# Attention batch 0 joined to a first MLP: the softmax constant as a column, the weights' low halves moved from GpSimd to VectorE

## Chip, cores, metric

One core of a Trainium2 chip runs the whole program. The metric is the device time of one execution in microseconds (us).

## What is computed

Pooled attention, then two MLPs on its output, in float32:

```
B, H, S, D = 8, 8, 576, 64          # Sp = S / 8 = 72
k_p = k.reshape(B, H, Sp, 8, D).mean(axis=3);  v_p = v.reshape(B, H, Sp, 8, D).mean(axis=3)
scores = (q @ k_p^T) / sqrt(D);  scores -= max(scores)
attn = exp(scores);  attn = attn / (sum(attn) + 1e-09)
x = (attn @ v_p) as 4608 x 512      # tokens x heads and head columns
h = relu(x @ w_in);   x = (h * h) @ w_out         # d_ff 2048
h = x @ w_in2;  g = h if h >= 1, 0 if h <= -1, else (h + 1)^2 / 4;  out = g @ w_out2
```

## The kernel before

Each float32 value of the MLPs is kept as a high part (rounded, `w_hi`) and a low part (the rest, `w_lo`), and every product is three matmul passes: high by high, high by low, low by high. Tokens go in nine chunks of 512 for each MLP. A chunk has 16 blocks f of 128 hidden columns: `hidden(f)` is twelve matmuls of 512 columns (4 blocks kd of the model width, 3 passes) into `ps_h`, then relu and square on ScalarE and VectorE with the split into `g_hl`, then `output(f)`, twelve matmuls into `ps_y`. `hidden` runs two blocks ahead of `output`. Attention of batch b+1 is done in slots between the matmuls of chunk b.

Batch 0 has nothing to hide behind, so the functions named `first_...` run it alone, ahead of chunk 0, as eight units u: head pair u // 2, half u % 2 of the queries. For one unit TensorE turns q (`first_turn_q`, L815) and for even u also pools and turns k; ScalarE copies both; TensorE makes scores (L833); VectorE takes maxima and subtracts them (`first_shift`, L681); ScalarE takes exp (L524); VectorE sums, adds the constant and multiplies by 8 in a 6-column TENSOR_SCALAR (L696) and takes the reciprocal; GpSimd scales (`first_scale`, L437); TensorE turns the probabilities (`first_turn_p`, L843); ScalarE copies them to `p_t` (L529), reordering columns; TensorE multiplies with v (`first_pv`, L857); ScalarE and VectorE split the result into x high and low (L534, L709). `keep_warm` (L810) is a matmul whose result nobody reads.

Every engine has its own order of instructions, written out by hand, and they meet only at semaphores. Around the end of batch 0:

- GpSimd adds up v (L421), scales units 0 to 6, subtracts the low halves of weight blocks 0 and 1 (`first_w_lo`, L442), then goes to batch 1's k (`pool_sum`, L447). Unit 7 is scaled by VectorE (`last_scale`, L703).
- ScalarE casts whole weight blocks of 1024 columns (`split_w`, L501; 512 of w_in, 512 of w_out) within units 5 to 7.
- TensorE runs the first matmuls of hidden blocks 0 and 1 between the last units (`first_hidden_hi`, `first_hidden_lo`, L936 and L944), then chunk 0.
- SP issues all loads in one queue; the load of weight block 4 waits until the staging slot of block 0 has been read.

```
            first_pv(NU - 3)
            pe.wait_ge(q_copied, NU - 1)
            first_hidden_hi(0, range(2))
            first_turn_p(NU - 2)
            first_pv(NU - 2)
            pe.wait_ge(shifted, NU - 1)
            first_hidden_hi(1, range(2))
            first_turn_p(NU - 1)
```

## Time and profile before

| | us |
|---|---|
| median of 3 runs | 1770.72 |
| lowest, highest | 1768.55, 1771.09 |
| the profiled execution | 1771.15 |
| its span, first to last instruction | 1769.4 |
| TensorE busy | 1751.3 (99%) |
| VectorE, ScalarE, GpSimd busy | 761.8, 553.7, 229.7 |

The profile is of one execution. TensorE's busy time counts pipelined matmuls, so it shows whether the engine had something to do, not how fast it did it. The stretch that the change touches is the first 55 us of the span. Idle time counts only where it holds TensorE up.

### The profile page before, as it was taken

To read this page: it belongs to the slowest core of one execution; us is meant where nothing else is said; L and a number is where in the kernel's file an instruction comes from. 1 tells how busy PE (TensorE), PEld (TensorE's weight loads), DVE (VectorE), ACT (ScalarE), POOL (GpSimd) and SP (SyncE) were. 2 spreads that over 40 slices of the span, in tenths; PEclk is the share of its full clock that TensorE was granted. 3 is DMA by queue.
4 is the path that set the end of the run, shared out by engine and by line. 5 is a ranking of instruction groups with operands and counts; after the bars stand their busy time and mean duration, and the time that the engine had idled before them with its cause. 6 is when DMAs were issued, how large, how long until landed. Compare 5 with 4: busy or idle time off the path is not lost.

```text
span 1769.4 us, 22412 instructions
## 1 busy us (share of the span) xinstructions
PE 1751.3 (99%) x8371; PEld 1413.9 (80%) x8371; DVE 761.8 (43%) x1211; ACT 553.7 (31%) x970; POOL 229.7 (13%) x254
## 2 busy tenths in 40 slices
PE   8999999999999999999999999999999999999999
PEld 6777777777777777778888788888888888888887
DVE  6664434444444443433235434343434343434343
ACT  5453333333333333332234322222222222222222
POOL 6332313223131231310000000000000000000000
PEclk8999999999999999999999999999999999999999
DMA  6453324242331423213035202020201020201000
GB/s 153 126 153 122 85 71 120 65 124 81 104 99 59 130 74 118 84 61 107 1 116 170 95 1 72 1 71 0 71 0 71 0 71 0 71 0 71 0 24 24
DMA packets 117062, 126.86 MB, mean 72 GB/s; under 512 B 40192, under 2 KB 72448, under 8 KB 116992
## 3 DMA queue, kind: packets, MB, share of 16 engines
q1 hardware_dynamic: 116992, 125.86, 23.1%
q8 instruction: 53, 0.87, 0.2%
q14 instruction: 17, 0.14, 0.0%
HBM read 80.74 MB, written 45.09 MB: 71 GB/s over the span
## 4 chain that ended last, share of the span: by engine, by line
PE 96%; DVE 2%; ACT 1%; issue 0%; DMA 0%; POOL 0%; SPq 0%; ACTq 0%
PE ps_h L931 44%; PE ps_y L968 44%; PE ps_a L882 2%; PE ps_a L906 2%; PE ps_a L919 2%; PE ps_a L896 1%; DVE sq_f L726 1%; DMA first_kv<-in_v 0%; PE ps_h L941 0%; ACT act_f L569 0%; PE ps_y L863 0%; PE ps_y L852 0%; DVE probs L664 0%; DVE stat L662 0%; POOL first_kv L434 0%
## 5 line engine op out<-in xcount | busy, mean ns | idle before, releaser
L931 PE MATMUL ps_h<-xc,w_hi 128*128 128x512 f32 x2288 | 715.1, 394 | 0.0
L931 PEld LDWEIGHTS ps_h<-xc,w_hi 128*128 128x128 f32 x2288 | 423.0, 188 | 93.4 <-issue 9.2
L931 PE MATMUL ps_h<-xc,w_lo 128*128 128x512 f32 x1144 | 446.7, 390 | 0.0
L968 PE MATMUL ps_y<-w_hi,g_hl 128*128 128x512 f32 x1152 | 379.6, 391 | 3.1 <-DVE stage L750 2.2
L968 PE MATMUL ps_y<-g_hl,w_hi 128*128 128x512 f32 x1152 | 366.3, 399 | 1.5 <-DVE g_hl L730 1.5
L726 DVE TENSOR_TENSOR sq_f<-act_f 128x512 f32<-128x512 f32 x144 | 111.4, 774 | 414.0 <-ACT act_f L569 414.0
L968 PEld LDWEIGHTS ps_y<-w_hi,g_hl 128*128 128x128 f32 x1152 | 217.1, 188 | 49.0 <-DVE stage L750 2.6
L968 PEld LDWEIGHTS ps_y<-g_hl,w_hi 128*128 128x128 f32 x1152 | 209.7, 188 | 57.2 <-issue 15.3
L576 ACT ACTIVATE act_f<-act_f,half_bias 128x512 f32<-128x512 f32 x144 | 104.2, 724 | 480.2 <-DVE act_f L737 480.2
L931 PEld LDWEIGHTS ps_h<-xc,w_lo 128*128 128x128 f32 x1144 | 214.5, 188 | 46.4
L968 PE MATMUL ps_y<-g_hl,w_lo 128*128 128x512 f32 x576 | 225.7, 392 | 0.0
L968 PE MATMUL ps_y<-w_lo,g_hl 128*128 128x512 f32 x576 | 224.6, 390 | 0.0
L737 DVE TENSOR_SCALAR act_f<-ps_h 128x512 f32<-128x512 f32 x144 | 99.4, 690 | 252.3 <-PE ps_h L931 252.3
L569 ACT ACTIVATE act_f<-ps_h 128x512 f32<-128x512 f32 x144 | 86.0, 597 | 365.1 <-PE ps_h L931 363.3
L740 DVE TENSOR_TENSOR act_f<-ps_h,act_f 128x512 f32<-128x512 f32 x144 | 99.5, 691 | 113.8 <-ACT act_f L576 113.8
L743 DVE TENSOR_TENSOR g_hl<-act_f,g_hl 128x512 fp32r<-128x512 f32 x144 | 99.6, 692 | 98.7 <-ACT g_hl L579 98.7
L453 POOL TENSOR_TENSOR kv_raw<-kv_raw 72x512 f32<-72x512 f32 x112 | 119.5, 1067 | 115.0 <-DMA kv_raw<-in_k 110.7
L968 PEld LDWEIGHTS ps_y<-g_hl,w_lo 128*128 128x128 f32 x576 | 108.1, 188 | 24.6
L968 PEld LDWEIGHTS ps_y<-w_lo,g_hl 128*128 128x128 f32 x576 | 108.5, 188 | 22.5
L579 ACT CAST g_hl<-act_f 128x512 fp32r<-128x512 f32 x144 | 89.3, 620 | 109.0 <-DVE act_f L740 109.0
L730 DVE TENSOR_TENSOR g_hl<-sq_f,g_hl 128x512 fp32r<-128x512 f32 x144 | 108.4, 753 | 6.2 <-DVE sq_f L726 0.4
L470 POOL TENSOR_TENSOR probs<-probs,stat 96x432 f32<-96x432 f32 x56 | 52.8, 942 | 386.7 <-DVE stat L679 386.7
(81 smaller groups left out, 945.9 us busy)
## 6 DMA issues: line engine op xcount, KB each, us to landing
mlp_out_hl<-stage SPq DMA_DIRECT2D x36, 512.0 KB, 4.3
xc<-mlp_out_hl SPq DMA_DIRECT2D x36, 512.0 KB, 5.7
xc<-attn_out_hl SPq DMA_DIRECT2D x32, 512.0 KB, 3.9
attn_out_hl<-xo_hl SPq DMA_DIRECT2D x56, 288.0 KB, 2.3
out<-stage SPq DMA_DIRECT2D x36, 256.0 KB, 2.1
stage<-in_moe_w_in SPq DMA_DIRECT2D x32, 256.0 KB, 3.6
stage<-in_moe_w_out SPq DMA_DIRECT2D x32, 256.0 KB, 4.7
kv_raw<-in_k SPq DMA_DIRECT2D x28, 288.0 KB
```

Of the source, the lines that this page charges most:

```text
L453: nc.gpsimd.tensor_tensor(raw[:, :, 0:width], raw[:, :, 0:width], raw[:, :, width:2 * width], ALU.add).then_inc(kv_add, 1)
L470: nc.gpsimd.tensor_tensor(groups(probs[:, u % 2, :]), groups(probs[:, u % 2, :]), row_stat(u % 2, 3), ALU.mult).then_inc(probs_ready, 1)
L569: nc.scalar.activation(act_f[:, f % 2, :], ps_h[:, f % 2, :], ACT.Relu).then_inc(relu_done, 1)
L576: nc.scalar.activation(act_f[:, f % 2, :], act_f[:, f % 2, :], ACT.Square, bias=half_bias[:, 0:1], scale=0.5).then_inc(ramp_done, 1)
L579: nc.scalar.copy(g_hl[:, f % 2, 0, :], act_f[:, f % 2, :]).then_inc(g_hi_done, 1)
L726: nc.vector.tensor_tensor(sq_f[:, f % 2, :], act_f[:, f % 2, :], act_f[:, f % 2, :], ALU.mult).then_inc(square_done, 1)
L730: nc.vector.tensor_tensor(g_hl[:, f % 2, 1, :], sq_f[:, f % 2, :], g_hl[:, f % 2, 0, :].bitcast(F32), ALU.subtract).then_inc(g_ready, 1)
L737: nc.vector.tensor_scalar(act_f[:, f % 2, :], ps_h[:, f % 2, :], 1.0, -1.0, ALU.min, ALU.max).then_inc(clip_done, 1)
L740: nc.vector.tensor_tensor(act_f[:, f % 2, :], ps_h[:, f % 2, :], act_f[:, f % 2, :], ALU.max).then_inc(bend_done, 1)
L743: nc.vector.tensor_tensor(g_hl[:, f % 2, 1, :], act_f[:, f % 2, :], g_hl[:, f % 2, 0, :].bitcast(F32), ALU.subtract).then_inc(g_ready, 1)
L931: mm = nc.tensor.matmul(ps_h[:, f % 2, :], left[:, f, kd * P:(kd + 1) * P], xc[:, buf, right, kd, :], start=(kd == 0 and n == 0), stop=(kd ...
L968: mm = nc.tensor.matmul(ps_y[:, m, :], left, right, start=(f == 0 and n == 0), stop=(f == NF - 1 and n == 2))
```

## The change

- The constant stands as a 73rd column in each group of `first_p`, written once by GpSimd; the sum on VectorE runs over 73 columns, and the TENSOR_SCALAR of the eight units of batch 0 is gone. The factor 1/8 goes into ScalarE's copy to `p_t`.
- TensorE's transposes of probabilities write PSUM with a step of three columns, and ScalarE's copy reads and writes straight on.
- GpSimd scales unit 0 ahead of the second v, scales unit 7 too, does no w_lo, and goes on to batch 1's k.
- w_hi and w_lo of weight blocks 0 to 2 are made in halves of 512 columns by ScalarE and VectorE, the w_in halves ahead of the w_out halves, counted in `w_first_hi` and `w_first`.
- k of head pair 0 is loaded ahead of q and pooled ahead of turning q; there is one warm-up matmul more in three places.
- TensorE's matmuls of hidden block 0 come ahead of `first_pv(5)`, those of block 1 ahead of `first_pv(6)`; the last block's passes are reordered; the first half of hidden block 2 comes ahead of `output(0)`.

```diff
-              nc.sbuf_tensor("first_p", [QT, 3, GRP * SP_], F32) as first_p):
+              nc.sbuf_tensor("first_p", [QT, 3, GRP, SP_ + 1], F32) as first_p):
...
-                if 4 <= n < 6:
-                    sp.wait_ge(w_first, n - 3)
-                elif n >= 6:
-                    sp.wait_ge(w_ready, n - 5)
+                if 4 <= n < 7:
+                    sp.wait_ge(w_first, n)
+                elif n >= 7:
+                    sp.wait_ge(w_ready, n - 6)
...
+            first_load_k(0)
             first_load_q(0)
-            first_load_k(0)
...
+            nc.gpsimd.memset(first_p[:, :, :, SP_:SP_ + 1], EPS).then_inc(eps_set, 1)
...
             def first_scale(u):
                 pool.wait_ge(recip_done, u + 1)
-                nc.gpsimd.tensor_tensor(groups(first_p[:, u % 3]), groups(first_p[:, u % 3]), row_stat(u % 2, 3),
+                nc.gpsimd.tensor_tensor(first_p[:, u % 3, :, 0:SP_], first_p[:, u % 3, :, 0:SP_], row_stat(u % 2, 3),
                                         ALU.mult).then_inc(first_probs, 1)
-
-            def first_w_lo(n):
-                pool.wait_ge(w_hi_done, n + 1)
-                nc.gpsimd.tensor_tensor(w_lo[:, n, :], stage[:, n, :], w_hi[:, n, :].bitcast(F32),
-                                        ALU.subtract).then_inc(w_first, 1)
...
-            for hp in range(2):
-                for i in range(3):
-                    first_add_v(hp, i)
+            for i in range(3):
+                first_add_v(0, i)
             first_scale(0)
+            first_add_v(1, 0)
             first_scale(1)
+            first_add_v(1, 1)
+            first_add_v(1, 2)
+            first_scale(2)
             first_add_v(2, 0)
-            first_scale(2)
+            first_scale(3)
             first_add_v(2, 1)
-            first_scale(3)
             first_add_v(2, 2)
+            first_scale(4)
             first_add_v(3, 0)
-            first_scale(4)
+            first_scale(5)
             first_add_v(3, 1)
-            first_scale(5)
             first_add_v(3, 2)
             first_scale(6)
-            first_w_lo(0)
-            first_w_lo(1)
+            first_scale(7)
...
+            def first_split_w(n, half):
+                part = slice(half * DM, (half + 1) * DM)
+                act.wait_ge(w_loaded[n], 2 * DMA)
+                nc.scalar.copy(w_hi[:, n, part], stage[:, n, part]).then_inc(w_first_hi, 1)
...
             def first_copy_q(u):
+                if u == 0:
+                    act.wait_ge(k_turned, 1)
+                    copy_k(first_q_bank(1))
                 act.wait_ge(q_turned, u + 1)
                 copy_q(first_q_bank(u))
-                if u % 2 == 0:
+                if u and u % 2 == 0:
                     act.wait_ge(k_turned, u // 2 + 1)
-                    copy_k(first_q_bank(u + 1))
+                    copy_k(first_q_bank(1))
...
             def first_copy_p(u):
                 act.wait_ge(probs_turned, u + 1)
-                nc.scalar.copy(p_t[:].rearrange("n a (p j) -> n a j p", j=NJ),
-                               ps_y[0:SP_, 0:2, 0:HALF].rearrange("n a (j p) -> n a j p", j=NJ)).then_inc(p_copied, 1)
+                nc.scalar.activation(p_t[:], ps_y[0:SP_, 0:2, 0:HALF], ACT.Copy, scale=1.0 / POOL).then_inc(p_copied, 1)
...
+                    if layer == 1 and c.at(0) and f == 0:
+                        first_split_w(2, 1)
...
-                if u >= 5:
-                    split_w(u - 5)
+                if u >= NU - 2:
+                    first_split_w(u - NU + 2, 0)
             first_x_hi(NU - 3)
             first_copy_p(NU - 2)
             first_x_hi(NU - 2)
             first_copy_p(NU - 1)
+            first_split_w(2, 0)
             first_x_hi(NU - 1)
+            for n in range(2):
+                first_split_w(n, 1)
...
-                                        ALU.add).then_inc(sum_done, 1)
+                if u == 0:
+                    dve.wait_ge(eps_set, 1)
+                nc.vector.tensor_reduce(stat[:, u % 2, 1, :], first_p[:, u % 3], AX_X, ALU.add).then_inc(sum_done, 1)
                 dve.wait_ge(sum_done, u + 1)
-                nc.vector.tensor_scalar(stat[:, u % 2, 2, :], stat[:, u % 2, 1, :], EPS, float(POOL),
-                                        ALU.add, ALU.mult).then_inc(eps_done, 1)
-                dve.wait_ge(eps_done, u + 1)
                 if u >= 2:
                     dve.wait_ge(first_probs, u - 1)
-                nc.vector.reciprocal(stat[:, u % 2, 3, :], stat[:, u % 2, 2, :]).then_inc(recip_done, 1)
-
-            def last_scale():
-                u = NU - 1
-                dve.wait_ge(recip_done, u + 1)
-                nc.vector.tensor_tensor(groups(first_p[:, u % 3]), groups(first_p[:, u % 3]), row_stat(u % 2, 3),
-                                        ALU.mult).then_inc(last_probs, 1)
+                nc.vector.reciprocal(stat[:, u % 2, 3, :], stat[:, u % 2, 1, :]).then_inc(recip_done, 1)
+
+            def first_w_lo(n, half):
+                part = slice(half * DM, (half + 1) * DM)
+                dve.wait_ge(w_first_hi, 3 * half + n + 1)
+                nc.vector.tensor_tensor(w_lo[:, n, part], stage[:, n, part], w_hi[:, n, part].bitcast(F32),
+                                        ALU.subtract).then_inc(w_first, 1)
...
+                    if layer == 1 and c.at(0) and f == 0:
+                        first_w_lo(2, 1)
...
-                if u >= 3:
+                if 3 <= u < NU - 1:
                     first_x_lo(u - 3)
             first_sums(NU - 1)
-            last_scale()
+            first_x_lo(NU - 4)
             first_x_lo(NU - 3)
+            first_w_lo(0, 0)
+            first_w_lo(1, 0)
             first_x_lo(NU - 2)
-            split_w(2)
+            first_w_lo(2, 0)
             first_x_lo(NU - 1)
+            first_w_lo(0, 1)
+            first_w_lo(1, 1)
...
-                if u == NU - 1:
-                    pe.wait_ge(last_probs, 1)
-                else:
-                    pe.wait_ge(first_probs, u + 1)
+                pe.wait_ge(first_probs, u + 1)
...
                 for a in range(2):
                     for j in range(NJ):
-                        mm = nc.tensor.transpose(ps_y[0:SP_, a, j * QT:(j + 1) * QT],
-                                                 first_p[:, u % 3, (2 * j + a) * SP_:(2 * j + a + 1) * SP_],
+                        mm = nc.tensor.transpose(ps_y[0:SP_, a, 0:HALF].rearrange("n (p j) -> n j p", j=NJ)[:, j, :],
+                                                 first_p[:, u % 3, 2 * j + a, 0:SP_],
                                                  ident[0:QT, 0:QT])
                 mm.then_inc(probs_turned, 1)
...
+            def first_hidden(f, left, right, blocks, start=False, stop=False):
+                for kd in blocks:
+                    mm = nc.tensor.matmul(ps_h[:, f, :], left[:, f, kd * P:(kd + 1) * P], xc[:, 0, right, kd, :],
+                                          start=(start and kd == blocks[0]), stop=stop)
+                if stop:
+                    mm.then_inc(h_ready, 1)
 
...
+                if c.at(0) and f < 3:
+                    pe.wait_ge(w_first, f + 4)
...
+                        hidden(c, buf, f + 2, weights, [2, 3] if fixed == 0 and f == 0 else range(KD))
...
+            first_pool_k(0)
             first_turn_q(0)
-            keep_warm(2)
+            keep_warm(3)
             first_scores(0)
             first_turn_q(1)
-            keep_warm(1)
+            keep_warm(2)
             for u in range(NU - 1):
                 first_scores(u + 1)
                 if u + 2 < NU:
                     first_turn_q(u + 2)
+                if u % 2 == 0 and u + 2 < NU:
+                    first_pool_k(u // 2 + 1)
                 if u < 2:
-                    keep_warm(2)
+                    keep_warm(2 + u)
                 if u >= 2:
                     first_pv(u - 2)
                 if u >= 1:
                     first_turn_p(u - 1)
+            pe.wait_ge(q_copied, NU - 1)
+            first_hidden_hi(0, [0, 1])
             first_pv(NU - 3)
-            pe.wait_ge(q_copied, NU - 1)
-            first_hidden_hi(0, range(2))
             first_turn_p(NU - 2)
+            pe.wait_ge(shifted, NU - 1)
+            first_hidden_hi(1, [0, 1])
             first_pv(NU - 2)
-            pe.wait_ge(shifted, NU - 1)
-            first_hidden_hi(1, range(2))
             first_turn_p(NU - 1)
             for f in range(2):
                 first_hidden_hi(f, [2])
             first_pv(NU - 1)
             for f in range(2):
-                first_hidden_lo(f, range(KD - 1))
-            for f in range(2):
-                first_hidden_hi(f, [KD - 1])
-                first_hidden_lo(f, [KD - 1])
+                first_hidden_lo(f, [0, 1, 2])
+            pe.wait_ge(x_hi_done, NU)
+            first_hidden(0, w_hi, 0, [KD - 1])
+            first_hidden(0, w_lo, 0, [KD - 1])
+            pe.wait_ge(x_split, NU)
+            first_hidden(0, w_hi, 1, [KD - 1], stop=True)
+            first_hidden(1, w_hi, 0, [KD - 1])
+            first_hidden(1, w_lo, 0, [KD - 1])
+            first_hidden(1, w_hi, 1, [KD - 1], stop=True)
+            pe.wait_ge(relu_done, 1)
+            hidden(At(0), 0, 2, 0, [0, 1])
```

GpSimd's start of batch 0, before (`first_kv` is raw v, `v_sum` its sum, `first_p` the probabilities of a unit):

```order
L434 TENSOR_TENSOR first_kv<-first_kv 72x2x256 [waits v_first0]
L434 TENSOR_TENSOR first_kv<-first_kv 72x2x128 [waits first_add]
L431 TENSOR_TENSOR v_sum<-first_kv 72x128 [waits first_add]
L434 TENSOR_TENSOR first_kv<-first_kv 72x2x256 [waits v_first1]
L434 TENSOR_TENSOR first_kv<-first_kv 72x2x128 [waits first_add]
L431 TENSOR_TENSOR v_sum<-first_kv 72x128 [waits first_add]
L439 TENSOR_TENSOR first_p<-first_p,stat 96x432 [waits recip_done] x2
L434 TENSOR_TENSOR first_kv<-first_kv 72x2x256 [waits v_first2]
L439 TENSOR_TENSOR first_p<-first_p,stat 96x432 [waits recip_done]
```

and of the change:

```order
L436 TENSOR_TENSOR first_kv<-first_kv 72x2x256 [waits v_first0]
L436 TENSOR_TENSOR first_kv<-first_kv 72x2x128 [waits first_add]
L433 TENSOR_TENSOR v_sum<-first_kv 72x128 [waits first_add]
L441 TENSOR_TENSOR first_p<-first_p,stat 96x6x72 [waits recip_done]
L436 TENSOR_TENSOR first_kv<-first_kv 72x2x256 [waits v_first1]
L441 TENSOR_TENSOR first_p<-first_p,stat 96x6x72 [waits recip_done]
L436 TENSOR_TENSOR first_kv<-first_kv 72x2x128 [waits first_add]
L433 TENSOR_TENSOR v_sum<-first_kv 72x128 [waits first_add]
L441 TENSOR_TENSOR first_p<-first_p,stat 96x6x72 [waits recip_done]
L436 TENSOR_TENSOR first_kv<-first_kv 72x2x256 [waits v_first2]
```

The first scaling moved ahead of the second v, and each further v's additions behind the scaling of an earlier unit.

VectorE from the sum of unit 7 to the first square, before (`xc` is x low, `xo_hl` its tail):

```order
L693 TENSOR_REDUCE stat<-first_p 96x6 [waits exp_done]
L696 TENSOR_SCALAR stat<-stat 96x6 [waits sum_done]
L701 RECIPROCAL stat<-stat 96x6 [waits first_probs,eps_done]
L706 TENSOR_TENSOR first_p<-first_p,stat 96x432 [waits recip_done]
L717 TENSOR_TENSOR xc<-ps_y,xc 128x224 [waits x_hi_done]
L719 TENSOR_TENSOR xo_hl<-ps_y,xo_hl 128x64
L713 TENSOR_TENSOR xc<-ps_y,xc 128x288 [waits x_hi_done]
L653 TENSOR_TENSOR w_lo<-stage,w_hi 128x1024 [waits w_hi_done]
L717 TENSOR_TENSOR xc<-ps_y,xc 128x224 [waits x_hi_done]
L719 TENSOR_TENSOR xo_hl<-ps_y,xo_hl 128x64
L726 TENSOR_TENSOR sq_f<-act_f 128x512 [waits relu_done]
```

and of the change:

```order
L705 TENSOR_REDUCE stat<-first_p 96x6 [waits exp_done]
L709 RECIPROCAL stat<-stat 96x6 [waits first_probs,sum_done]
L721 TENSOR_TENSOR xc<-ps_y,xc 128x288 [waits x_hi_done]
L725 TENSOR_TENSOR xc<-ps_y,xc 128x224 [waits x_hi_done]
L727 TENSOR_TENSOR xo_hl<-ps_y,xo_hl 128x64
L714 TENSOR_TENSOR w_lo<-stage,w_hi 128x512 [waits w_first_hi] x2
L721 TENSOR_TENSOR xc<-ps_y,xc 128x288 [waits x_hi_done]
L714 TENSOR_TENSOR w_lo<-stage,w_hi 128x512 [waits w_first_hi]
L725 TENSOR_TENSOR xc<-ps_y,xc 128x224 [waits x_hi_done]
L727 TENSOR_TENSOR xo_hl<-ps_y,xo_hl 128x64
L714 TENSOR_TENSOR w_lo<-stage,w_hi 128x512 [waits w_first_hi] x2
L734 TENSOR_TENSOR sq_f<-act_f 128x512 [waits relu_done]
```

The TENSOR_SCALAR and the last scaling are gone, and five half subtractions of w_lo stand where one whole one stood.

TensorE at units 5 to 7, before (L863 and L875 are v products, L852 and L864 transposes of probabilities):

```order
L863 MATMUL ps_y<-p_t,v_sum 64x288 [waits x_split,first_v_pooled,p_copied]
L863 MATMUL ps_y<-p_t,v_sum 64x288
L941 MATMUL ps_h<-xc,w_hi 128x512 [waits x_split,w_hi_done,q_copied]
L941 MATMUL ps_h<-xc,w_hi 128x512
L852 MATMUL ps_y<-ident,first_p 72x96 [waits p_copied,first_probs]
L852 MATMUL ps_y<-ident,first_p 72x96 x5
L863 MATMUL ps_y<-p_t,v_sum 64x288 [waits x_split,first_v_pooled,p_copied]
L863 MATMUL ps_y<-p_t,v_sum 64x288
L941 MATMUL ps_h<-xc,w_hi 128x512 [waits x_split,w_hi_done,shifted]
```

and of the change:

```order
L864 MATMUL ps_y<-ident,first_p 72x96 [waits p_copied,first_probs]
L864 MATMUL ps_y<-ident,first_p 72x96 x5
L952 MATMUL ps_h<-xc,w_hi 128x512 [waits x_split,w_first_hi,q_copied]
L952 MATMUL ps_h<-xc,w_hi 128x512 x3
L875 MATMUL ps_y<-p_t,v_sum 64x288 [waits x_split,first_v_pooled,p_copied]
L875 MATMUL ps_y<-p_t,v_sum 64x288
L864 MATMUL ps_y<-ident,first_p 72x96 [waits p_copied,first_probs]
L864 MATMUL ps_y<-ident,first_p 72x96 x5
L952 MATMUL ps_h<-xc,w_hi 128x512 [waits x_split,w_first_hi,shifted]
```

The four w_hi matmuls of hidden block 0 moved ahead of the product of unit 5, block 1's ahead of that of unit 6.

## Rows read from the trace of the kernel before

**Rows 1.** The page: TensorE's busy time and share, and the chain by engine.
```profile
PE 1751.3 (99%) x8371; PEld 1413.9 (80%) x8371; DVE 761.8 (43%) x1211; ACT 553.7 (31%) x970; POOL 229.7 (13%) x254
...
PE 96%; DVE 2%; ACT 1%; issue 0%; DMA 0%; POOL 0%; SPq 0%; ACTq 0%
```

**Rows 2.** TensorE's timeline: start us, us, engine, line, operation, idle before and releaser.
```profile
14.77 0.73 PE L812 MATMUL ps_y<-warm 128*128 128x512 f32 x2
16.63 0.69 PE L852 MATMUL ps_y<-ident,first_p 96*72 96x96 f32 x6 [1.12 <-POOL first_p L439]
...
22.61 0.69 PE L852 MATMUL ps_y<-ident,first_p 96*72 96x96 f32 x6
...
28.59 0.69 PE L852 MATMUL ps_y<-ident,first_p 96*72 96x96 f32 x6
29.11 0.90 PE L839 MATMUL ps_a<-k_bd,q_t 128*96 128x144 f32 x6
30.79 0.71 PE L863 MATMUL ps_y<-p_t,v_sum 72*64 72x288 f32 x4 [0.78 <-ACT p_t L531]
...
33.25 1.23 PE L863 MATMUL ps_y<-p_t,v_sum 72*64 72x288 f32 x4 [1.13 <-ACT p_t L531]
...
38.46 1.23 PE L863 MATMUL ps_y<-p_t,v_sum 72*64 72x288 f32 x4 [1.01 <-ACT p_t L531]
...
49.12 0.73 PE L968 MATMUL ps_y<-g_hl,w_hi 128*128 128x512 f32 x2 [1.46 <-DVE g_hl L730]
...
66.75 0.66 PE L919 MATMUL ps_a<-ident,probs 96*72 96x96 f32 x6 [1.44 <-DVE probs L664]
```

**Rows 3.** Windows: busy of PE, PEld, DVE, ACT, POOL; granted clock; DMA; GB/s.
```profile
29.00:33.00 4.00, 2.34 (x20) 1.45 (x17) 3.49 (x11) 4.00 (x8) 1.69 (x3) 1.00 0.45 93
33.00:43.50 10.50, 9.24 (x31) 5.92 (x32) 8.07 (x8) 4.12 (x8) 10.27 (x8) 0.51 0.04 9
```

**Rows 4.** GpSimd's timeline, 13 to 66 us.
```profile
13.10 2.07 POOL L434 TENSOR_TENSOR first_kv<-first_kv 72x512 f32<-72x512 f32 x2
...
15.67 0.91 POOL L439 TENSOR_TENSOR first_p<-first_p,stat 96x432 f32<-96x432 f32 x1
...
33.50 4.68 POOL L444 TENSOR_TENSOR w_lo<-stage,w_hi 128x1024 fp32r<-128x1024 f32 x2
...
40.54 1.57 POOL L460 TENSOR_TENSOR k_sum<-kv_raw 72x128 f32<-72x128 f32 x1
...
52.36 0.46 POOL L460 TENSOR_TENSOR k_sum<-kv_raw 72x128 f32<-72x128 f32 x1 [8.21 <-PE ps_a L892]
62.30 0.91 POOL L470 TENSOR_TENSOR probs<-probs,stat 96x432 f32<-96x432 f32 x1 [9.48 <-DVE stat L679]
63.17 2.86 POOL L453 TENSOR_TENSOR kv_raw<-kv_raw 72x512 f32<-72x512 f32 x2
```

**Rows 5.** VectorE's timeline, 34 to 66 us.
```profile
34.26 3.95 DVE L696 TENSOR_SCALAR stat<-stat 96x6 f32<-96x6 f32 x1
...
47.64 0.69 DVE L726 TENSOR_TENSOR sq_f<-act_f 128x512 f32<-128x512 f32 x1 [1.88 <-ACT act_f L569]
...
62.47 1.28 DVE L726 TENSOR_TENSOR sq_f<-act_f 128x512 f32<-128x512 f32 x1 [0.25 <-ACT act_f L569]
63.79 1.66 DVE L730 TENSOR_TENSOR g_hl<-sq_f,g_hl 128x512 fp32r<-128x512 f32 x1
```

**Rows 6.** ScalarE's groups by shape: count | busy us, mean ns | idle before.
```profile
L579 ACT CAST g_hl<-act_f 128x512 fp32r<-128x512 f32 x144 | 89.3, 620 | 109.0 <-DVE act_f L740 109.0
...
L564 ACT COPY p_t<-ps_a 72x576 f32<-72x576 f32 x56 | 35.2, 629 | 22.7 <-PE ps_a L919 22.7
...
L531 ACT COPY p_t<-ps_y 72x576 f32<-72x576 f32 x8 | 7.6, 948 | 7.7 <-PE ps_y L852 7.5
```

**Rows 7.** TensorE's weight loads, timeline at 6 us.
```profile
6.07 1.07 PEld L828 LDWEIGHTS ps_a<-ident,first_kv 72*64 72x64 f32 x32 [0.42 <-DMA first_kv<-in_k]
```

**Rows 8.** The chain that ended last, in order of time: start us, us, what.
```profile
55.98 2.77 PE ps_y L968 x12
```

61 lines of the change are left out of this document (28 added, 33 removed).

## The prediction

> **What bounds the kernel now.** I read the busy shares first: TensorE is busy 1751.3 of 1769.4 us and makes up 96% of the chain that ended last [rows 1]. So nothing that another engine does counts unless TensorE waits for it. Then TensorE's timeline over the first 70 us, looking for gaps [rows 2]. Batch 0's attention has three parts. Up to 16.63 us it fills; the first transposes of probabilities start then, 1.12 us late, waiting for GpSimd. From 16.63 to 29.8 us TensorE has no gap: two units (u = 2, 3) take 28.59 - 22.61 = 5.98 us whatever the others do. From 29.85 us on it drains, with gaps of 0.78, 1.13, 1.01 and 1.46 us until the first product of the output matmul starts at 49.12. The only gap behind that in chunk 0 that I find is 1.44 us at 66.75. The windows [rows 3] show the second loss of the drain: between 29 and 33 us TensorE is busy 2.34 of 4 us at full clock, and from 33.0 to 43.5 us the granted clock is 0.51, the lower level (1.2 GHz). It fell after the gaps of 0.78 and 1.13 us, and rose once the matmuls stood close again.
>
> The cause on the other engines: VectorE's 6-column TENSOR_SCALAR at 34.26 takes 3.95 us [rows 5], exactly until GpSimd ends its two w_lo subtractions, 33.50 to 38.18 [rows 4]. The last unit's probabilities stand behind it. ScalarE meanwhile copies p_t in 0.95 us a time [rows 6], between w_hi casts of 1024 columns.
>
> **The start.** GpSimd ends batch 0's first v at 13.10 to 13.14 us, but starts the scaling of unit 0 only at 15.67, behind the second v [rows 4]. Now it scales at once: done at 13.14 + 0.91 = 14.05. Then TensorE itself decides: its two warm-ups at 14.77 end issue at 14.77 + 2 x 0.23 = 15.23, and the change adds one, 15.46. The loads give something back: k's first matmul waited at 6.07 for its load, with q already turned [rows 7]; now k is loaded and pooled first, and q, the last to land, is followed by 0.65 us of turning and 0.40 of copying instead of 1.17 and 0.45. That is worth 0 to 0.6 us; I take 0.3, since q's pieces may land a little after k's did. The other added warm-up stands in a wait for ScalarE's copy, so it costs nothing; if that copy were early it would cost 0.23. First transposes at 15.16 instead of 16.63: **1.47 us**. The close stretch carries this shift unchanged. On GpSimd the second v now ends near 17.8, and its first reader (unit 2's product) starts near 23.
>
> **The drain**, laid out by hand from the rows, all at full clock. Transposes of unit 4 at 27.12 (28.59 before). Steps on TensorE: 0.52 us for six transposes (28.59 to 29.11), 0.84 for scores and 0.55 for a pv pair (busy 0.90 and 0.71, less the overlap with what follows [rows 2]), 0.23 for a matmul of 512 columns (twelve take 2.77 [rows 8]). On ScalarE p_t's copy is now contiguous: 0.65 instead of 0.95, after the 0.63 of batch 1's same copy [rows 6]; a w_hi half is 0.60, after the 0.62 of a cast of 512 columns [rows 6]. On VectorE the constant as a 73rd column removes the TENSOR_SCALAR (0.17 to 3.95 us) from all eight units. pv(4) starts at 28.54 and transposes(5) at 29.10; the four w_hi matmuls of block 0 now stand between them and pv(5) and fill the gap: 29.62 to 30.56. pv(5) 30.56. Transposes(6) need exp(6) 29.03, sum 30.34, reciprocal 30.53, scaling by GpSimd 31.49: start 31.54, a gap of 0.43. Block 1's four matmuls 32.06 (before 39.62), pv(6) 32.99, transposes(7) 33.54, scaling(7) by GpSimd having ended at 32.85. Then four w_hi matmuls 34.06, pv(7) 34.99, six w_lo 35.54, and the last six to 38.3. Relu(0) 37.84 to 38.44. The first half of hidden block 2 (six matmuls, 1.39 us), formerly behind the first output, fills 38.49 to 39.88.
>
> **What the moved work costs.** Five half w_lo subtractions and GpSimd's batch-1 additions now fall between 32.8 and 42 us. Where a TENSOR_TENSOR of VectorE meets a GpSimd instruction, the rows show one waiting for the other: the square at 62.47 takes 1.28 instead of 0.69 while GpSimd scales until 63.2; the subtraction at 63.79 takes 1.66 while GpSimd adds; and GpSimd's k_sum takes 1.57 instead of 0.46 under VectorE's w_lo [rows 4, 5]. They take turns. With additions of 1.26 and 0.80 (2.07 a pair), 0.46, and 1.26 and 0.80 again [rows 4], in turn with halves of 0.66 us (a little under the 0.69 of a square of 512 columns [rows 5]): w_lo(0) is ready at 33.5, w_lo(1) 35.4 (needed 36.2), w_lo(2) 36.9 (needed 38.5), output half 0 at 38.0, output half 1 at 39.9. Then square(0) waits out GpSimd's last addition, 40.73, and ends at 41.42, g_lo(0) at 42.11: first output matmul at 42.16. Without any turns, g_lo(0) would come at 38.49 + 0.69 + 0.72 = 39.9 and the output at 40.0. So the turns cost 2.2 us there, in the largest wait left.
> The Trainium skill (SBUF — State Buffer, section Who interferes with whom) says that a VectorE instruction with two SBUF inputs contends with a GpSimd instruction that reads SBUF, the first holding the port for its whole length, and that a reduce never does. It speaks against moving w_lo to VectorE without a hold on GpSimd; the traced 1.28, 1.66 and 1.57 us agree, and the reduces and reciprocals keep their length.
>
> **Sum.** The first output starts at 42.16 instead of 49.12, 6.96 us earlier (1.47 from the start, 5.49 from the drain), with 1.39 us of hidden block 2 already done: **8.35 us**. From there the same work follows in the same order. The wait at 66.75 comes from scores, maxima and the square held by GpSimd, all counted from TensorE's own start of output(1), so it should stay. Loads of weights 4 to 6 now wait for w_first, ready from 38.0 on, and SP reaches them only behind the x stores, which wait for unit 7's x split, now 37.3: nothing. The kernel's own profiled execution took 1771.15 us (span 1769.4): 1762.8. The median shown is 0.43 lower, 1770.72, so the forecast is **1762.4 us**.
>
> **Unknown prices.** ScalarE's copy with a factor: 0.63 to 0.95 us [rows 6]; at 0.95 the first output is at 42.76, 0.6 us later. Transposes that write PSUM with a step of three: no row has it. From below nothing, or a little less; from above, the nearest row is ScalarE's stepped copy, 0.95/0.63 = 1.5 times, which on 0.52 us for eight units is 2.1 us. I take nothing, since the step changes no count of columns, and keep 2.1 for the range. Turns between the two engines: from 0 (first output near 40.0, 2.2 us more gain) to the hold below.
>
> **The rivals.**
> 1. *The clock still falls in the drain* (0.14). For: it fell before after gaps of 0.78 and 1.13 us, and one of some 2.1 us stays in front of the first output. Against: every other gap is at most 0.43, and the 1.46 us gap before 49.12 came at full clock. If it ran at the lower level over the whole 30 to 40 us, some 5 us of matmuls would take twice as long: gain 3.4, 1767.4. If only behind the last gap, 2 to 3 us are lost: 1765.
> 2. *The hold comes back in another form* (0.12): GpSimd's additions follow one another as its two w_lo did, and VectorE is held over all five (4.6 us, to 38.1). For: the 3.95 us. Against: the additions wait for each other and let VectorE in (63.17 to 66.03). w_lo(1) at 38.7, first output near 42.9: 1763.2.
> 3. *The start gives nothing* (0.08): q lands later, or a load after it, and TensorE reaches unit 0's transposes only at 16.6: 1763.9.
> 4. *The stepped PSUM write is dear* (0.12), the case on the other side. It stands in the close stretch, where each of 48 transposes counts. At k times the price the loss is 4.2 (k - 1) us: 1764.5 at 1.5 times; at 3 times (a step of three costing what the span of columns does) the whole gain is gone, 1770.8; beyond 3.9 times it is slower than now by over 0.2%. For: ScalarE pays for a step. Against: TensorE passes columns one by one.
>
> **How the numbers follow.** The forecast has 0.54; its own range is 1760.0 (no turns) to 1764.5. 0.2% is 3.5 us, about what a measurement tells here. Faster by more: forecast 0.54, hold 0.12, start 0.08, clock 0.10 of 0.14, stepped write 0.04 of 0.12: 0.88. Within: 0.04 + 0.03 = 0.07. Slower: 0.05. The range, 1759.5 to 1767.0, reaches over the hold, the start and most of the clock, and leaves out the dear write and a drain wholly at the lower clock.
>
> **What would show it.** Right: first transposes of p near 15.2; no TENSOR_SCALAR on VectorE before batch 1; granted clock 1.0 throughout 33 to 43; p_t copies of 0.65; w_lo halves up to 1.9 us long beside GpSimd; six L944 matmuls before the first output, and that output near 42.2 behind a wait of about 2 us for g_hl. Wrong: six transposes over 0.6 us (rival 4), a clock row under 1 (rival 1), a w_lo half over 3 us (rival 2), first transposes at 16.6 (rival 3), or a gap behind the first output larger than the 1.44 us at 66.75.

## The result, and the profile after

| us | before | after |
|---|---|---|
| median (lowest, highest; executions) | 1770.89 (1768.55, 1772.47; 8) | 1763.77 (1762.58, 1765.52; 8) |
| profiled execution, its span | 1771.15, 1769.4 | 1764.07, 1762.3 |
| TensorE busy | 1751.3 | 1747.7 |

The change makes the kernel 0.4% faster: ratio 0.9962, 95% interval [0.9953, 0.9971], 7.1 us by the medians. The forecast was 1762.4 us, 1.4 us too low; the range of 1759.5 to 1767.0 holds the result.

The page of the kernel after, TensorE's busy time and the chain by engine, to be put beside [rows 1]:

```profile
PE 1747.7 (99%) x8374; PEld 1411.7 (80%) x8374; DVE 760.3 (43%) x1207; ACT 552.0 (31%) x973; POOL 226.6 (13%) x254
...
PE 97%; DVE 2%; issue 0%; ACT 0%; POOL 0%; ACTq 0%; POOLq 0%
```

TensorE's timeline of the kernel after (start us, us, engine, line, operation, count, idle before and releaser), to be put beside [rows 2]:

```profile
15.42 0.66 PE L864 MATMUL ps_y<-ident,first_p 96*72 96x96 f32 x6
...
27.35 0.69 PE L864 MATMUL ps_y<-ident,first_p 96*72 96x96 f32 x6
...
29.89 1.17 PE L952 MATMUL ps_h<-xc,w_hi 128*128 128x512 f32 x4
30.99 0.71 PE L875 MATMUL ps_y<-p_t,v_sum 72*64 72x288 f32 x4
31.84 0.69 PE L864 MATMUL ps_y<-ident,first_p 96*72 96x96 f32 x6
...
34.04 0.69 PE L864 MATMUL ps_y<-ident,first_p 96*72 96x96 f32 x6
...
39.29 0.73 PE L944 MATMUL ps_h<-xc,w_hi 128*128 128x512 f32 x2
...
41.39 0.70 PE L985 MATMUL ps_y<-g_hl,w_hi 128*128 128x512 f32 x2 [0.44 <-DVE g_hl L738]
...
57.62 0.66 PE L931 MATMUL ps_a<-ident,probs 96*72 96x96 f32 x6 [1.44 <-DVE probs L674]
...
383.75 0.66 PE L931 MATMUL ps_a<-ident,probs 96*72 96x96 f32 x6 [1.35 <-DVE probs L674]
```

Windows of the kernel after (busy of PE, PEld, DVE, ACT, POOL; granted clock; DMA; GB/s), to be put beside [rows 3]:

```profile
29.00:33.00 4.00, 3.86 (x27) 2.40 (x24) 3.42 (x10) 3.48 (x9) 3.16 (x5) 1.00 0.21 51
33.00:43.50 10.50, 10.05 (x48) 6.58 (x47) 9.95 (x14) 7.08 (x14) 6.13 (x6) 1.00 0.22 65
```

The drain is closed: the w_hi matmuls of block 0 (29.89) stand where TensorE waited 1.13 us, the granted clock is 1.00 where it was 0.51, and TensorE waits 0.44 us in front of the first output. The row at 57.62 is the same work as the one at 66.75 in [rows 2], with the same wait of 1.44 us. By there 66.75 - 57.62 = **9.13 us** are gained: 1.21 in front of the first transposes of p (16.63 against 15.42), and 7.92 between the two marks (50.12 us before, 42.20 after). I call this stretch, from the first transposes of p to batch 1's first transposes of probs, the **drain mark**. The end has only 1771.15 - 1764.07 = 7.08 us of the 9.13: **2.05 us are given back later**, in two steps. Against the same rows of before, the kernel after is 9.09 us ahead at its row at 274.69, 8.29 at the one at 383.75, where the wait is 1.35 us instead of 0.59, 7.03 at the one at 601.58, and between 7.02 and 7.08 from there to the end.

GpSimd's timeline of the kernel after, beside [rows 4]:

```profile
12.96 0.90 POOL L441 TENSOR_TENSOR first_p<-first_p,stat 96x432 f32<-96x432 f32 x1
...
33.05 2.86 POOL L450 TENSOR_TENSOR kv_raw<-kv_raw 72x512 f32<-72x512 f32 x2
35.99 0.97 POOL L457 TENSOR_TENSOR k_sum<-kv_raw 72x128 f32<-72x128 f32 x1
36.93 2.44 POOL L450 TENSOR_TENSOR kv_raw<-kv_raw 72x512 f32<-72x512 f32 x2
```

VectorE's timeline of the kernel after, beside [rows 5]:

```profile
32.79 2.53 DVE L714 TENSOR_TENSOR w_lo<-stage,w_hi 128x512 fp32r<-128x512 f32 x2
...
37.38 2.53 DVE L714 TENSOR_TENSOR w_lo<-stage,w_hi 128x512 fp32r<-128x512 f32 x2
39.84 0.68 DVE L734 TENSOR_TENSOR sq_f<-act_f 128x512 f32<-128x512 f32 x1
...
374.52 0.69 DVE L734 TENSOR_TENSOR sq_f<-act_f 128x512 f32<-128x512 f32 x1 [5.60 <-issue]
```

The scaling of unit 0 starts right behind the first v (12.96). Pairs of w_lo halves take 2.53 us beside the additions. The last row is new: 5.60 us in which VectorE waited for nothing that the profile shows; the square at the same place before, at 382.06, stands behind ScalarE's relu (4.40 us idle). The page's rows for the queues of instruction fetches (queue: packets, MB, share), first of before, then of after:

```profile
q14 instruction: 17, 0.14, 0.0%
```

```profile
q14 instruction: 27, 0.22, 0.0%
```

The ten more packets all lie between 367 and 800 us, five from 367 on and five from 583 on, at the loop's two ways back; before has none there.

### The profile page after: what moved, and what is told of

Read it like the earlier page. It is cut to its first block, busy times and chain, and to the rows that moved or that the text cites. A ratio compares the mean times of both kernels' runs of the same rounds, so it can differ in the third digit from the quotient of the medians.

```text
span 1762.3 us, 22444 instructions
## 1 busy us (share of the span) xinstructions
PE 1747.7 (99%) x8374; PEld 1411.7 (80%) x8374; DVE 760.3 (43%) x1207; ACT 552.0 (31%) x973; POOL 226.6 (13%) x254
## 4 chain that ended last, share of the span: by engine, by line
PE 97%; DVE 2%; issue 0%; ACT 0%; POOL 0%; ACTq 0%; POOLq 0%
PE ps_h L944 44%; PE ps_y L985 44%; PE ps_a L894 2%; PE ps_a L918 2%; PE ps_a L931 2%; PE ps_a L908 1%; DVE sq_f L734 1%; PE ps_y L826 0%; PE ps_a L843 0%; DVE probs L674 0%; PE ps_y L864 0%; ACT act_f L574 0%; DVE stat L672 0%; PE ps_y L875 0%; PE ps_h L854 0%
```

## The experiments

How they compare: how long TensorE's first matmuls run at half rate differs from execution to execution (last section) and moves everything behind them by up to 2.7 us, so single profiles are compared by the drain mark, and times by the ratio to the kernel before on the same chip. The three chips are those of a_body226, a_pad4, b_body234 and b_column; of a_pvfirst, a_hold, b_hifirst and b_colhi; and of b_wvec, b_wvechi, a_vfirst and a_nohid2. Medians of two chips are not compared closely.

One thing more moves the times, whatever the kernel. In front of the second MLP, near 980 us, TensorE waits 2.17 us in every profile. Behind this wait the granted clock falls for about 3.4 us in 12 of the 14 profiled executions, and not in those of a_body226 and a_nohid2; from there to the end TensorE takes 778.0 us with the fall (after: 977.95 to 1755.96) and 776.5 without (a_body226: 977.68 to 1754.14). Windows of after and of a_body226:

```profile
977.50:982.50 5.00, 4.55 (x13) 3.60 (x14) 3.53 (x7) 2.48 (x5) 0.00 (x0) 0.66 0.75 277
```

```profile
977.50:982.50 5.00, 4.82 (x21) 3.98 (x22) 3.52 (x7) 2.22 (x4) 0.00 (x0) 1.00 0.81 297
```

Of an execution without a profile only the mean granted clock over the whole kernel is known. In the profiled ones it is 0.996 with before's fall in the drain and this one (10 and 3 us), 0.998 with a fall of about 3.5 us in each place (b_hifirst), 0.999 with one fall of some 3 us, and 1.000 with none (a_body226).

| kernel | median us | ratio, 95% interval | first p | drain mark |
|---|---|---|---|---|
| before | 1770.7, 1771.3, 1771.6 (three chips) | | 16.63 | 50.12 |
| after | 1763.77 | 0.9962 [0.9953, 0.9971] | 15.42 | 42.20 |
| a_body226 | 1761.24 | 0.9950 [0.9937, 0.9962] | 17.34 | 42.24 |
| a_pad4 | 1763.21 | 0.9963 [0.9948, 0.9977] | 14.80 | 42.19 |
| a_pvfirst | 1763.58 | 0.9957 [0.9944, 0.9970] | 14.74 | 43.21 |
| a_hold | 1762.85 | 0.9952 [0.9938, 0.9966] | 17.42 | 42.71 |
| a_vfirst | 1763.16 | 0.9953 [0.9940, 0.9967] | 16.89 | 42.26 |
| a_nohid2 | 1763.63 | 0.9955 [0.9941, 0.9969] | 17.43 | 45.16 |
| b_body234 | 1771.97 | 1.0004 [0.9995, 1.0013] | 17.07 | 50.07 |
| b_column | 1771.04 | 0.9996 [0.9985, 1.0007] | 15.86 | 49.94 |
| b_hifirst | 1771.19 | 1.0001 [0.9992, 1.0011] | 16.53 | 49.19 |
| b_colhi | 1769.59 | 0.9989 [0.9977, 1.0000] | 18.44 | 49.33 |
| b_wvec | 1767.47 | 0.9979 [0.9970, 0.9988] | 16.67 | 46.58 |
| b_wvechi | 1765.73 | 0.9968 [0.9955, 0.9980] | 16.85 | 44.95 |

### Where 2 us went: the length of VectorE's loop

The diff touches one line of VectorE inside the loop: `b.times(NU, u + 1)` became `b.times(NU, u + 1 - NU)`, since batch 0 no longer counts eps_done. That value was shared with other waits; now it needs register instructions of its own. Counted in the program, the loop over chunks has 226 instructions on VectorE before and 234 after.

**a_body226**: the changed kernel, with the constant's memset counting for batch 0.

```diff
-            nc.gpsimd.memset(first_p[:, :, :, SP_:SP_ + 1], EPS).then_inc(eps_set, 1)
+            nc.gpsimd.memset(first_p[:, :, :, SP_:SP_ + 1], EPS).then_inc(eps_done, NU)
-                    dve.wait_ge(eps_set, 1)
+                    dve.wait_ge(eps_done, NU)
-                    dve.wait_ge(eps_done, b.times(NU, u + 1 - NU))
+                    dve.wait_ge(eps_done, b.times(NU, u + 1))
```

> The changed kernel, but the memset of the constant's column counts eps_done up to 8, so that the wait of batches 1 to 7 is again on the same register value as the others and the loop of VectorE has 226 instructions as before the change, instead of 234 (its start stays at instruction 152). Theory 1 (the longer loop body no longer fits what VectorE keeps, so its start is fetched again at each way back): the two late starts of VectorE at the second and third pass (5.60 us before the square at 374.5) are gone, the waits of TensorE there are 0.59 instead of 1.35, and the kernel is 1.6 to 2.2 us faster than the change: 1761.7. Theory 2 (the position of the loop's start, which the change moved from instruction 156 to 152): no difference, 1763.8. Theory 3 (the stores beside it slow the same fetch): no difference.

TensorE's timeline of a_body226 at the place of the row at 383.75, and its page's row for the fetches:

```profile
384.86 0.66 PE L930 MATMUL ps_a<-ident,probs 96*72 96x96 f32 x6 [0.59 <-DVE probs L673]
```

```profile
q14 instruction: 17, 0.14, 0.0%
```

The wait is back at 0.59 us, the fetches at 17, and the time is 1761.24 us: 9.5 us under before's median on that chip. Not all of the 2.5 us to after's median is the loop's: four of the six executions have a mean clock of 1.000 (1759.75 to 1762.22 us), the other two, with 0.999 like all eight of after, took 1762.49 and 1764.65. What the loop costs is read from the traces. **a_pad4** keeps 234 instructions and moves where the loop starts, by four memsets of one column ahead of it on VectorE:

```diff
+            for i in range(4):
+                nc.vector.memset(pad[:, i:i + 1], 0.0)
```

> The changed kernel with four memsets of one column each ahead of everything on VectorE, where it idles for 8 us: the loop starts at instruction 156 again, as before the change, and keeps its 234 instructions. Theory 1 (length of the body): the two late starts stay, 1763.8. Theory 2 (position of the start): they are gone, 1761.7.

It stays near after's time, with 27 fetch packets, as theory 1 had it; only the places moved (TensorE waits 0.33 and 1.32 us for the late q_t at 378.68 and 596.44). The waits of a_pad4, VectorE's (engine, line waited for: us in total, times, longest):

```profile
DVE g_hl L739 <- issue: 6.2, 2, 3.5
```

**b_body234** is the reverse: the kernel before, batch 0 counting on a semaphore of its own.

```diff
-                                        ALU.add, ALU.mult).then_inc(eps_done, 1)
-                dve.wait_ge(eps_done, u + 1)
+                                        ALU.add, ALU.mult).then_inc(eps_first, 1)
+                dve.wait_ge(eps_first, u + 1)
...
-                    dve.wait_ge(eps_done, b.times(NU, u + 1))
+                    dve.wait_ge(eps_done, b.times(NU, u + 1 - NU))
```

> The kernel before, with batch 0's TENSOR_SCALAR counted in a semaphore of its own, so that the loop of VectorE has 234 instructions instead of 226 and starts at 156 as before; nothing else. Theory 1: the two late starts appear here too and cost 1.6 to 2.2 us: 1772.7. Theory 2: no difference, 1770.8.

VectorE's waits in b_body234:

```profile
DVE stat L663 <- issue: 5.6, 2, 3.0
```

The late starts come, at the two ways back of the loop, with 27 packets, and TensorE waits 0.94 and 0.34 us for q_t there; the median is 1.2 us above before's, which its interval can't tell from nothing. The traces can: from batch 1's first transposes of probs to those of batch 7 (66.75 to 716.94 in before) TensorE takes 652.30, 651.66 and 651.43 us in the three kernels with 234 instructions, and 649.90 to 650.58 in ten of the eleven with 226; the eleventh, a_pvfirst, has 651.19, with 0.82 us of TensorE's own `issue` idle. So the eight instructions are the cause of the late starts in both kernels, and they cost 1 to 2 us, by what TensorE needs from VectorE just then. The Trainium skill (Runtime: NRT & Kernel Launch, section Instruction fetch mechanics) says that an engine's instruction memory holds two blocks, filled in sequence, and that a taken branch to a target outside of them waits for a fetch. The ten added packets and the 5.60 us at the loop's way back agree; that the step from 226 to 234 crosses such an edge is my reading, and no run measured where the edge lies.

### What closed the drain: the change in parts, on the kernel before

**b_column**: the constant as a column, with the factor in ScalarE's copy, and nothing else.

```diff
-                nc.vector.tensor_scalar(stat[:, u % 2, 2, :], stat[:, u % 2, 1, :], EPS, float(POOL),
-                                        ALU.add, ALU.mult).then_inc(eps_done, 1)
-                dve.wait_ge(eps_done, u + 1)
```

> The kernel before with the constant as a column alone: no TENSOR_SCALAR in batch 0, the factor 1/8 in ScalarE's copy (which still reorders columns), all orders as before, GpSimd's w_lo too. Theory A (the prediction's: VectorE's instruction held for 3.95 us is what makes the drain long): unit 7's probabilities come up to 3 us earlier and the first output starts 2 to 4 us earlier, 1767 to 1769. Theory B (it stood in the shadow of TensorE at the lower clock and of ScalarE's copies; unit 7's transposes at 41.49 waited for the matmuls ahead of them, not for the probabilities ready at 39.9): the first output moves by less than 0.5 us, 1770.5.

VectorE's timeline of b_column:

```profile
33.48 0.19 DVE L701 RECIPROCAL stat<-stat 96x6 f32<-96x6 f32 x1
33.70 3.97 DVE L706 TENSOR_TENSOR first_p<-first_p,stat 96x432 f32<-96x432 f32 x1
```

The held instruction is gone, and the next one is held in its stead, 3.97 us for 3.95, over GpSimd's w_lo subtractions (32.54 to 37.21). The reciprocal, which starts beside them too, takes its usual 0.19. The column alone is worth nothing beyond the start: theory B. The median hides two of the ten executions, 1765.68 and 1765.92 us, whose mean clock of 1.000 leaves room for neither of the two falls.

**b_hifirst**: the order of TensorE alone. **b_colhi**: both.

```diff
-            first_pv(NU - 3)
             pe.wait_ge(q_copied, NU - 1)
             first_hidden_hi(0, range(2))
+            first_pv(NU - 3)
...
-            first_pv(NU - 2)
             pe.wait_ge(shifted, NU - 1)
             first_hidden_hi(1, range(2))
+            first_pv(NU - 2)
```

> The kernel before with one thing of the change: the four w_hi matmuls of block 0 ahead of pv(5), those of block 1 ahead of pv(6). Theory 'order': the gaps of 1.13 and 1.01 us fill, units 5 and 6 come about 1 us each earlier; the transposes of unit 7 then wait in the open for VectorE's TENSOR_SCALAR held to 38.2 and its scaling to 39.9 (now 41.5): 1.6 to 2 us gained at full clock, and the wait of some 3.9 us shows as a gap. If the clock stays full up to there, what it costs (about 5 us, from the two runs of b_column that kept it) comes on top in part: 1764 to 1766; if the clock falls in the long gap instead, 1768 to 1769. Theory 'VectorE decides': no more than 1.6 us.

> The kernel before with the constant as a column (b_column) and the w_hi matmuls ahead of pv(5) and pv(6). In b_column the hold had passed from the TENSOR_SCALAR to the next instruction, the last scaling (TENSOR_TENSOR, 3.97 us, to 37.67), so that the column gained nothing but the start. Against b_hifirst the column now saves the TENSOR_SCALAR and the reciprocal behind the hold, 0.8 us of start and about 1.4 us of the scaling: unit 7's transposes at 37.7 instead of 39.9, 2 us more gained than b_hifirst (1762 to 1766). If w_lo on VectorE is what counts, the gap of 1.8 us in front of unit 7 stays, and the time stays 1.5 us or more above that of a_body226 (1761.2).

TensorE's timeline of b_hifirst:

```profile
35.67 0.71 PE L863 MATMUL ps_y<-p_t,v_sum 72*64 72x288 f32 x4 [0.23 <-ACT p_t L531]
39.84 1.07 PE L852 MATMUL ps_y<-ident,first_p 96*72 96x96 f32 x6 [3.46 <-DVE first_p L706]
40.62 2.05 PE L941 MATMUL ps_h<-xc,w_hi 128*128 128x512 f32 x4
```

The gaps of 1.13 and 1.01 us shrink to 0.17 and 0.23, and what they hid appears: one gap of 3.46 us for unit 7's probabilities, behind the held TENSOR_SCALAR. The clock falls behind it (four w_hi matmuls in 2.05 us; 1.17 in front of it), and nothing is left of the gain: 0.93 us at the drain mark, none in the median. In b_colhi the gap is 2.02 us, the clock falls all the same, and 1.7 us are gained by the median, at the edge of its interval. For b_hifirst the theory "VectorE decides" held; the 1762 to 1766 expected of b_colhi missed, and its other theory, that w_lo on VectorE is what counts, is the one that fits.

**b_wvec**: w_lo(0) and w_lo(1) on VectorE, nothing else. **b_wvechi**: that and the order of b_hifirst.

```diff
-                pool.wait_ge(w_hi_done, n + 1)
-                nc.gpsimd.tensor_tensor(w_lo[:, n, :], stage[:, n, :], w_hi[:, n, :].bitcast(F32),
+                dve.wait_ge(w_hi_done, n + 1)
+                nc.vector.tensor_tensor(w_lo[:, n, :], stage[:, n, :], w_hi[:, n, :].bitcast(F32),
...
             first_x_lo(NU - 3)
+            first_w_lo(0)
             first_x_lo(NU - 2)
+            first_w_lo(1)
             split_w(2)
```

> The kernel before with one thing of the change: w_lo(0) and w_lo(1) made by VectorE (whole, 1024 columns) and not by GpSimd, behind the last scaling and the split of unit 5's x; TensorE's order and the constant as before. Theory 'both together': the hold on the TENSOR_SCALAR (3.95 us) goes, but the gaps of 0.78 and 1.13 us in front of pv(4) and pv(5) stay, so the clock falls at about 33 us as before, and unit 7 comes only as far ahead as the doubled durations let it: gain 0 to 1 us, 1770.3 to 1771.3. Theory 'the hold was it': unit 7 comes as soon as its probabilities are there, the clock rises earlier: 2 to 4 us gained, 1767 to 1769.

> The kernel before with two things of the change: w_lo(0) and w_lo(1) on VectorE as in b_wvec, and the w_hi matmuls ahead of pv(5) and pv(6) as in b_hifirst. Theory 'both together': no gap over 0.8 us up to the last matmul of hidden block 1, granted clock 1.0 throughout, unit 7's transposes at about 36.3 instead of 39.8 in b_hifirst; the first output some 5 to 6 us ahead of before's: 1765 to 1766.5, below the sum of the two alone. Theory 'the column is needed too' (its TENSOR_SCALAR and reciprocal and the last scaling on VectorE stay in front of unit 7): under 3 us, 1768 or more.

TensorE's timeline of b_wvec:

```profile
30.85 0.71 PE L863 MATMUL ps_y<-p_t,v_sum 72*64 72x288 f32 x4 [0.79 <-ACT p_t L524]
...
33.30 0.71 PE L863 MATMUL ps_y<-p_t,v_sum 72*64 72x288 f32 x4 [1.13 <-ACT p_t L524]
33.94 1.20 PE L941 MATMUL ps_h<-xc,w_hi 128*128 128x512 f32 x4
...
36.65 0.71 PE L863 MATMUL ps_y<-p_t,v_sum 72*64 72x288 f32 x4 [1.02 <-ACT p_t L524]
```

Its windows, and VectorE's TENSOR_SCALAR of unit 7:

```profile
33.00:43.50 10.50, 8.86 (x46) 5.61 (x47) 8.43 (x12) 4.68 (x10) 7.65 (x6) 1.00 0.06 13
```

```profile
34.31 0.54 DVE L689 TENSOR_SCALAR stat<-stat 96x6 f32<-96x6 f32 x1
```

This part alone gives 4.1 of the 7.1 us: theory "the hold was it" (1767 to 1769), and not the 0 to 1 us of the other; but the clock didn't rise earlier in this profile, it never fell in the drain. The TENSOR_SCALAR takes 0.54 us, unit 7's scaling ends at 36.09 instead of 39.87, and TensorE goes through the **same three gaps** as before (0.79, 1.13, 1.02 us) with the clock at 1.00. A mean clock of 0.999 or more over the whole kernel, which leaves no room for before's fall of 10 us, stands in 9 of its 11 executions, and in 9 of the 64 of the kernel before (1 of 16 on the same chip). The two others of b_wvec took 1770.91 and 1771.61 us, hardly less than before's 1771.66 with the fall on that chip: the gain comes where the clock is kept. With the order on top the drain mark falls by another 1.63 us, and the median stands 5.9 us below before's, as "both together" had it; the order alone was worth nothing. So the parts don't add up one by one: the order pays once the hold on VectorE is gone, and the hold goes only with w_lo off GpSimd.

What else lies between b_wvechi (44.95) and after (42.20) is 2.75 us: 1.39 of it the half of hidden block 2, the rest the column, the contiguous copy, and w_lo in halves, which were not tried apart on this base.

### The parts taken out of the changed kernel

These four stand on a_body226. **a_pvfirst** puts pv(5) and pv(6) back in front of the w_hi matmuls:

```diff
-            first_hidden_hi(0, [0, 1])
             first_pv(NU - 3)
+            first_hidden_hi(0, [0, 1])
...
+            first_pv(NU - 2)
             pe.wait_ge(shifted, NU - 1)
             first_hidden_hi(1, [0, 1])
-            first_pv(NU - 2)
```

> The changed kernel with a_body226's form of the semaphore (so that the loop keeps its 226 instructions), and on TensorE the old order alone: pv(5) and pv(6) each ahead of the four w_hi matmuls that the change put in front of them. Theory 'order': these eight matmuls fill the waits for p_t's copy (TensorE has no gap over 0.2 us between 29 and 38 us in the changed kernel), and that keeps the granted clock at full. With the old order two gaps of 0.6 to 1.1 us come back (start times alone: about 1.2 to 1.5 us, 1762.6) and, if gaps decide the clock as in the kernel before, it falls to about 0.5 behind them, and costs some 5 us more: 1766 to 1768. Theory 'VectorE': what let the clock fall was the late last unit, behind GpSimd's w_lo; the order is worth its 1.2 to 1.5 us only, the clock stays 1.0: 1762.4 to 1762.8.

TensorE's timeline and a window of a_pvfirst:

```profile
30.21 0.71 PE L874 MATMUL ps_y<-p_t,v_sum 72*64 72x288 f32 x4 [0.78 <-issue]
...
33.27 0.71 PE L874 MATMUL ps_y<-p_t,v_sum 72*64 72x288 f32 x4 [0.74 <-ACT p_t L536]
```

```profile
33.00:43.50 10.50, 10.22 (x48) 7.02 (x49) 7.82 (x13) 7.09 (x14) 4.91 (x5) 1.00 0.22 65
```

Two gaps come back, cost 0.97 us at the drain mark, and the clock stays at 1.00 in this profile; none of the seven executions has a mean under 0.999, so none had a fall of 10 us. The order is worth its own gaps, and is not what holds the clock here: theory "VectorE" of the two, though its 1762.4 to 1762.8 was 1 us low.

**a_hold** gives GpSimd the hold that the change leaves out:

```diff
             first_scale(7)
+            pool.wait_ge(w_first, 5)
```

> The changed kernel with a_body226's form of the semaphore, and GpSimd waits for all five halves of w_lo of VectorE (w_first 5) before it goes on to batch 1's k. Theory of the prediction: the turns with GpSimd's additions cost 2.2 us in front of the first output; without them VectorE's pairs of w_lo take 1.4 instead of 2.53 us, the wait of TensorE in front of the first output goes, and the time falls by up to 2 us: 1759.2. Theory from the trace of after: only 0.44 us of TensorE's wait is left there, so at most 0.4 us is gained (1760.8); the additions, now from about 40.6 us on, meet the squares and g_lo instead, and may give that back and up to 1 us more (1762.2). Batch 1's k_sum at about 43 us stays ahead of TensorE's transpose of it (46 us).

VectorE's timeline of a_hold, and TensorE's first output:

```profile
39.39 1.29 DVE L714 TENSOR_TENSOR w_lo<-stage,w_hi 128x512 fp32r<-128x512 f32 x2
41.28 1.32 DVE L734 TENSOR_TENSOR sq_f<-act_f 128x512 f32<-128x512 f32 x1 [0.59 <-ACT act_f L574]
42.64 1.11 DVE L738 TENSOR_TENSOR g_hl<-sq_f,g_hl 128x512 fp32r<-128x512 f32 x1
```

```profile
43.89 0.70 PE L985 MATMUL ps_y<-g_hl,w_hi 128*128 128x512 f32 x2 [0.93 <-DVE g_hl L738]
```

The pair of halves takes 1.29 us alone instead of 2.53, but ends before relu(0) does, so that nothing is gained from it; the square and g_lo then meet the additions, 1.32 and 1.11 us instead of 0.68 and 0.69. The wait in front of the first output grows from 0.44 to 0.93, the drain mark by 0.47. In these two traces going on without a hold is right, by half a microsecond, and the turns in front of the first output cost at most 0.44 us. The median, 1762.85, lies above both forecasts; the ratios of the two kernels differ by 0.0002, far inside their intervals.

**a_vfirst** puts both first v ahead of the scaling of unit 0 on GpSimd again, as before:

```diff
-            first_scale(0)
-            first_add_v(1, 0)
-            first_scale(1)
-            first_add_v(1, 1)
-            first_add_v(1, 2)
+            for i in range(3):
+                first_add_v(1, i)
+            first_scale(0)
+            first_scale(1)
```

> The changed kernel with a_body226's form of the semaphore, and GpSimd's start as before: both first v ahead of the scaling of unit 0. Theory of the prediction: the scaling's place is what gives the start's gain, the first transposes of p wait 1.1 to 1.5 us again, and all behind them is that much later: 1762.3 to 1762.7 (a_body226: 1761.24). Rival: TensorE's own first 10 us, at half rate in some executions up to 10 us, make it reach the first transposes only at 17.3 us in those, so there GpSimd's order costs nothing, and over many executions less than half of it shows: 1761.3 to 1761.8.

TensorE's first transposes of p in a_vfirst:

```profile
16.89 0.69 PE L862 MATMUL ps_y<-ident,first_p 96*72 96x96 f32 x6 [1.30 <-POOL first_p L440]
```

In this execution TensorE's first microseconds are those of the profile of after (k's pooling 1.89 us in both), and the first transposes come 1.47 us later. The drain mark is unchanged (42.26). By the ratios it costs 0.0003, about 0.5 us, which is inside both intervals and decides between neither theory; the median lies above both (1763.16), but its 1.9 us to a_body226's are of two chips.

**a_nohid2** leaves hidden block 2 whole behind the first output:

```diff
-            pe.wait_ge(relu_done, 1)
-            hidden(At(0), 0, 2, 0, [0, 1])
...
-                        hidden(c, buf, f + 2, weights, [2, 3] if fixed == 0 and f == 0 else range(KD))
+                        hidden(c, buf, f + 2, weights)
```

> The changed kernel with a_body226's form of the semaphore, and hidden block 2 whole behind the first output, as before. Theory of the prediction: its first six matmuls (1.39 us) stand in a wait for g_hl and are a full gain; without them TensorE waits 0.44 + 1.39 = 1.83 us in front of the first output, which starts as now, and the rest is 1.39 us later: 1762.6. Rival: what follows waits for VectorE further on (the 1.44 us at 57.6 us of the changed kernel), and takes up the 1.39: 1761.2.

TensorE's timeline of a_nohid2:

```profile
43.40 0.70 PE L984 MATMUL ps_y<-g_hl,w_hi 128*128 128x512 f32 x2 [2.10 <-DVE g_hl L737]
...
45.07 1.05 PE L984 MATMUL ps_y<-g_hl,w_hi 128*128 128x512 f32 x2
```

The first output starts where it does in a_body226 (43.33), and the drain mark is 2.92 us longer: the 1.39 us of the six matmuls, and some 1.5 us because the granted clock fell behind the wait of 2.10 us (0.50 from 45 to 48). The median is 1 us above the 1762.6 of the first theory; against the rival speaks the trace, in which nothing up to batch 1 takes up the 1.39 us. So the half block fills a wait; that it also keeps the engine at its clock rests on this one profile. One of the five executions has a mean clock of 1.000 (1761.75 us), so the clock doesn't fall there each time.

## Why the prediction was right, and where it was off

- **Direction and size: right.** 8.35 us forecast, 7.08 measured between the two profiled executions.
- **The start**, 1.47 us forecast, 1.21 measured. GpSimd's scaling was out of the way as forecast; a_vfirst undoes this part and its first transposes come 1.47 us later at the same pace of TensorE's start. At the slower pace of a_body226 TensorE itself reaches them only at 17.34, so the gain isn't there in every execution. The 0.3 us hoped from loading k first went another way: q's turning was to take 0.65 us and k's pooling to lie ahead of it, but the pooling ran partly at half rate, 1.89 us for 1.22. In a_pad4, where it took 1.22, the first transposes came at 14.80.
- **The close stretch** carried the shift: transposes of unit 4 at 27.35, 11.93 us behind the first ones; 11.96 before.
- **The drain up to hidden block 2**: the rows follow the hand-made schedule with small additions (pv(5) 30.99 for 30.56, transposes of unit 7 at 34.04 for 33.54, block 2 at 39.29 for 38.49). Counted from the first transposes that is 0.54 us later than forecast.
- **The turns with GpSimd: oversized.** "The turns cost 2.2 us there": at most 0.44 are left. I let the engines strictly take turns, so that GpSimd's last addition ended at 40.73 and square(0) waited for it. It ended at 39.37, for two additions beside two halves take 2.86 and 2.44 us, not the sum of 2.08 and 1.29. The first output came at 41.39 for 42.16, with 0.44 us of waiting in front of it instead of about 2. From the start of hidden block 2 to the first output the forecast has 3.67 us and the trace 2.10, so this term hid 1.57 us of gain; less the 0.26 of the start and the 0.54 above, the gain at the first output was 0.77 us larger than forecast.
- **Hidden block 2's half, 1.39 us: right**, and a_nohid2's profile adds a fall of the clock without it, about 1.5 us.
- **"From there the same work follows in the same order": this step failed.** The work is the same, VectorE's instructions are not: eight more register instructions in the loop, two late starts, 2.05 us. The diff shows the line, and the prediction took a changed wait value as costing nothing. With the value put back (a_body226) the median is 1761.24, 1.2 us under the forecast. So the 1.3 us between 8.35 and 7.08 are no measure of how good the sum was: two misses, 0.77 us too little up to the first output and 2.05 us too much behind it, partly cancelled, and that is luck.
- **The cause named for the drain**: the TENSOR_SCALAR of 3.95 us. Half right. The hold is there, but it is no property of that instruction: take it out and the next is held (b_column). What removes it is w_lo leaving GpSimd (b_wvec), and that is worth 4.1 us, most of it where the clock is kept; that the hold is what takes the clock away isn't shown.
- **"It fell after the gaps of 0.78 and 1.13 us"**: as a description right, as an explanation it doesn't hold alone. b_wvec has the same gaps and keeps the clock in its profile, and 9 of its 11 executions have a mean clock of 0.999 or more.
- **The rivals.** Clock falls: no, 1.00 in both windows, and in a_pvfirst too. The hold in another form: no VectorE instruction near it; the longest pair 2.53 us. The start gives nothing: no. The stepped PSUM write is dear: no, six transposes 0.66 to 0.69 us as before. ScalarE's copy with the factor took 0.65 us, as taken:

```profile
L537 ACT ACTIVATE p_t<-ps_y 72x576 f32<-72x576 f32 x8 | 5.2, 647 | 2.4 <-PE ps_y L864 2.3
```

**What stays open.** Before, the clock falls at about 33.3 us, nearly one microsecond before the hold on VectorE begins (34.26), and from the first transposes of p (16.63) up to there TensorE's rows in b_wvec are the same within 0.06 us. Yet the mean clock is 0.999 or more in 9 of 64 executions of one kernel and in 9 of 11 of the other. Either the fall depends on something that the profile doesn't show, or in most executions of b_wvec it comes and is short, since unit 7 is there early. One profile of each can't tell. It also isn't shown how the gain of b_wvec divides into clock and waits. As an estimate from the means: before's nine executions with 0.999 have a median of 1768.5 us, the 55 others 1771.7, and b_wvec's nine have 1767.2, so about 3 us would be the clock's and about 1 the hold's.

## What to carry to other kernels

A loop's length in instructions was a resource here: before a wait inside a hardware loop is given a new register value, count the instructions of the body on that engine, and look for `issue` idle at the loop's way back and for added instruction packets in the page. When several engines are late in one place, taking out the instruction that shows the long time may only hand the hold to its neighbour, as in b_column; take out what it collides with, and try orders and gap fillers again after that. A filler in a wait of the bounding engine gave its own time here (1.39 us), and in one profile the rate of what follows too.

## What the runs showed of the hardware

- **A hold passes on.** VectorE's TENSOR_SCALAR on 6 columns took 3.95 us beside two GpSimd subtractions, and a TENSOR_TENSOR in its place 3.97. It goes the other way too: in b_wvechi GpSimd's k_sum, 0.46 us in other places, took 4.91 us beside seven VectorE instructions, three whole w_lo among them.

```profile
35.89 4.91 POOL L455 TENSOR_TENSOR k_sum<-kv_raw 72x128 f32<-72x128 f32 x1
```

- **TensorE's first microseconds differ between executions.** The same 32 matmuls that pool k, in a_pad4 and in a_body226:

```profile
4.67 1.22 PE L846 MATMUL ps_a<-ident,first_kv 72*64 72x72 f32 x32
```

```profile
4.72 2.19 PE L842 MATMUL ps_a<-ident,first_kv 72*64 72x72 f32 x32
```

In the second the half rate lasts to about 10.5 us, and the first transposes come at 17.34 instead of 14.80, though the column of the granted clock reads 1.00 in both. This is part of the spread of the changed kernels (up to 5.3 us), with the fall in front of the second MLP that comes or doesn't, and hides half-microsecond effects: a_vfirst's 1.47 us and b_body234's 1.3 us showed in the traces, and hardly in the ratios.
- **What a gap does to the clock isn't fixed by its length.** 1.13 us: it fell before, not in b_wvec. 3.46 and 2.02 us: it fell (b_hifirst, b_colhi). 2.10 us in front of the first output: it fell for some 3 us (a_nohid2). 2.17 us in front of the second MLP: it fell in 12 of 14 profiles. 0.93 and 1.44 us: it didn't (a_hold; and all profiles at batch 1).
